# Windowed attention and two expert layers: another order for attention's first steps

## The reference

```
attention (2 batches, 8 heads, 768 positions, 64 wide):
  scores = q k^T / 8;  kept where key < n_sink or 0 <= query - key < window, else -1e9
  a = exp(scores - rowmax);  a /= sum(a) + 1e-9;  x = a v        -> 1536 x 512
expert layer 1: logits = x w_gate + modality_bias[modality_id]; the best of 8 experts per row,
  out = softmax weight * relu(x w1[e]) w2[e]
expert layer 2: all 8 experts, mixed by a table that is normalised over rows and columns 8 times
```

## Time and profile before

| | us |
|---|---|
| median of 3 runs | 1458.73 (1458.69 to 1463.12) |
| profiled execution, its own time | 1461.2 |
| its span | 1459.4 |
| granted TensorE clock, mean | 0.987 |
| PE busy | 1419.9 (97%) |
| DVE, ACT, POOL busy | 515.5, 355.8, 229.6 |
| attention | from 0 to about 149.8 |
| its part in which PE isn't yet without gaps | from 0 to 51.1 |

### The profile page before, as it was taken

The page is one execution under the profiler, slowest core; times in us unless marked ns, Lnnn a source line. Parts: engine busy times, 40 slices in busy tenths (PEclk is TensorE's granted clock), DMA queues, the critical chain, the costliest instruction groups (busy, mean ns, idle before and its releaser), DMA issues.

```text
span 1459.4 us, 18534 instructions
## 1 busy us (share of the span) xinstructions
PE 1419.9 (97%) x7023; PEld 1183.5 (81%) x7024; DVE 515.5 (35%) x935; ACT 355.8 (24%) x627; POOL 229.6 (16%) x252
## 2 busy tenths in 40 slices
PE   8999989999589999999999999999999999999999
PEld 7999678888458888888888888888888888888887
DVE  7887662232453222222222222222222222222222
ACT  4887432322221111121111111121111112121100
POOL 2111022222221111120211111120211111120200
PEclk9999999999799999999999999999999999999999
DMA  5442371121400000000101000000101000010001
GB/s 105 101 96 59 124 260 57 43 101 43 151 29 30 29 29 30 29 29 29 57 0 57 29 29 29 29 29 29 57 0 57 29 29 29 29 34 25 0 20 67
DMA packets 70461, 74.40 MB, mean 51 GB/s; under 512 B 42640, under 2 KB 42640, under 8 KB 70416
## 3 DMA queue, kind: packets, MB, share of 16 engines
q1 hardware_dynamic: 64800, 65.35, 14.2%
q0 software_dynamic: 2576, 8.39, 1.7%
q10 hardware_dynamic: 3040, 0.06, 0.1%
HBM read 63.30 MB, written 10.49 MB: 51 GB/s over the span
## 4 chain that ended last, share of the span: by engine, by line
PE 92%; DVE 4%; issue 2%; DMA 1%; POOL 1%; ACT 0%; SPq 0%; POOLq 0%; DVEq 0%
PE ps L1761 36%; PE ps L1731 35%; PE ps L1629 6%; PE ps L1651 5%; PE ps L1446 2%; PE ps L1375 1%; PE ps L1405 1%; PE ps L1638 1%; PE ps L1563 1%; PE ps L1388 1%; PE ps L1440 1%; PE ps L1360 1%; POOL wsplit L670 1%; DMA v_all<-in_v_dram 1%; PE ps L1609 0%
## 5 line engine op out<-in xcount | busy, mean ns | idle before, releaser
L1731 PE MATMUL ps<-x_hi,wsplit 128*128 128x512 f32 x1536 | 484.1, 390 | 1.4 <-DVE x_lo L1266 1.4
L1761 PE MATMUL ps<-wsplit,h_hi 128*128 128x512 f32 x1536 | 474.6, 390 | 0.0
L1731 PEld LDWEIGHTS ps<-x_hi,wsplit 128*128 128x128 f32 x1536 | 289.1, 188 | 61.6 <-DVE x_lo L1266 1.8
L1761 PEld LDWEIGHTS ps<-wsplit,h_hi 128*128 128x128 f32 x1536 | 289.1, 188 | 59.8
L847 ACT ACTIVATE h_hi<-ps 128x512 fp32r<-128x512 f32 x192 | 114.8, 598 | 866.8 <-PE ps L1731 866.8
L1761 PE MATMUL ps<-wsplit,h_lo 128*128 128x512 f32 x768 | 299.5, 390 | 0.0
L1731 PE MATMUL ps<-x_lo,wsplit 128*128 128x512 f32 x768 | 299.3, 390 | 0.0
L670 POOL TENSOR_TENSOR wsplit<-stage,wsplit 128x2048 fp32r<-128x2048 f32 x32 | 147.1, 4598 | 820.6 <-ACT wsplit L843 820.6
L1289 DVE SCALAR_TENSOR_TENSOR h_lo<-ps,h_hi 128x512 fp32r<-128x512 f32 x192 | 132.7, 691 | 404.9 <-ACT h_hi L847 404.7
L1331 DVE SCALAR_TENSOR_TENSOR acc<-ps,mix,acc 128x512 f32<-128x512 f32 x192 | 143.9, 750 | 347.9 <-PE ps L1761 347.9
L1761 PEld LDWEIGHTS ps<-wsplit,h_lo 128*128 128x128 f32 x768 | 144.6, 188 | 30.1
(11 more groups left out here) (239 smaller groups left out, 979.6 us busy)
## 6 DMA issues: line engine op xcount, KB each, us to landing
stage<-in_moe_w_dram SPq DMA_DIRECT2D x40, 1024.0 KB, 5.2
first_raw<-in_moe_w_dram SPq DMA_DIRECT2D x4, 1024.0 KB, 7.9
q_raw<-in_q_dram SPq DMA_DIRECT2D x12, 256.0 KB, 3.3
k_raw<-in_k_dram SPq DMA_DIRECT2D x12, 256.0 KB, 4.2
v_all<-in_v_dram SPq DMA_DIRECT2D x12, 256.0 KB, 4.6
x_rows_dram<-x_rows SPq DMA_DIRECT2D x12, 256.0 KB, 3.6
y_rows<-y_rows_dram SPq DMA_DIRECT2D x12, 256.0 KB, 4.8
out_dram<-acc SPq DMA_DIRECT2D x12, 256.0 KB, 2.0
```

Source lines behind the costliest of these rows:

```text
L1731: last = pe.matmul(ps[:, f, :], w_part[:, ws], x_part[:, kc, toks], start=(kc == 0 and n == 0), stop=(kc == KD - 1 and n == 2))
L1761: last = pe.matmul(ps[:, 4 + t, :], h_part[:, s % 2, kc, ts], w_part[:, ks], start=(kc == 0 and n == 0), stop=(kc == 3 and n == 2))
```

## The change

It does six things.

1. The six small loads get two semaphores: scalars_loaded for n_sink and window, small_loaded for the other four. DVE waits for the scalars only; the others are waited for where they are used.
2. v gets a semaphore for each tile; a tile's q and k no longer share theirs with v. SP issues q, k of tile 0, the sink keys, q, k of tile 1, then v of both tiles. DVE zeroes v_sink first.
3. DVE makes the masks (with the caps of tiles 0 and 1) before it splits half 0.
4. The sinks' keys are copied once from PSUM into an SBUF table sink_keys, from there in two copies to k_cur (zeroed by a memset), and in four copies to k_sink after masking step 1. POOL waits for these on a semaphore of their own, and copies v of tile 0 first.
5. q and k are transposed, evacuated and split four steps ahead instead of three: a fourth `transpose_qk` and `qk_evacuate` stand in the start, and the loop does step c + 4.
6. In the first iteration, PE transposes step 0's probabilities and runs 8 keep_busy transposes before the scores of step 2; the string before the flag grows from 14 to 20.

```diff
@@ SP
             load_tile(1)
+            load_values(0)
+            load_values(1)
             sp.wait_ge(sinks_zeroed, 1)
...
                 load_tile(m)
+                load_values(m)
@@ POOL, attention_copies
+                def copy_values(t):
+                    pool.wait_ge(v_loaded[2 * i + t], 16)
+                    if not (first_pair and t == 0):
+                        pool.wait_ge(pv_done, lin(i, 4, 2 * t))
+                    hold(2 + t)
+                    pool.tensor_tensor(v_use[:, t, :], v_all_flat[:, bass.ds(lin(i, 2 * DM, t * DM), DM)], ones_row,
+                                       ALU.mult).then_inc(v_ready, 1)
+                if first_pair:
+                    copy_values(0)
...
+                        if first_pair and t == 0:
+                            pool.wait_ge(sinks_copied, 1)
                         pool.wait_ge(scores_done, lin(i, 4, 2 * t + 2))
...
-            pool.wait_ge(sinks_ready, 3)
@@ ACT
-            for c in range(3):
+            for c in range(4):
                 qk_evacuate(0, c)
...
+                    if begin and c == 0:
+                        p_evacuate(i, c)
                     if not (final and c + 1 >= 4):
                         exps(i, c + 1)
-                    if not (final and c + 3 >= 4):
-                        qk_evacuate(i, c + 3)
-                    p_evacuate(i, c)
+                    if not final:
+                        qk_evacuate(i, c + 4)
+                    if not (begin and c == 0):
+                        p_evacuate(i, c)
@@ DVE
+            dve.memset(v_sink[:, :, :, :], 0.0).then_inc(sinks_zeroed, 1)
+            dve.memset(k_cur[:, :, :, :], 0.0).then_inc(k_cur_begun, 1)
...
-            dve.wait_ge(small_loaded, 16 * 6)
+            dve.wait_ge(scalars_loaded, 16 * 2)
             dve.wait_ge(consts_ready, 3)
...
             link(dve.tensor_scalar(sinkcap[:, :, :], sinkcap[:, :, :], KEEP - MASKED, MASKED, ALU.mult, ALU.add))
+            caps(0)
+            caps(1)
+
+            qk_lo(0, 0)
+
+            dve.wait_ge(sinks_ready, 1)
+            dve.tensor_copy(sink_keys[:, :], ps[:, 5, 0:2 * 4 * SINKS]).then_inc(sinks_ready, 1)
+            dve.wait_ge(sinks_ready, 2)
+            dve.wait_ge(k_cur_begun, 1)
+            for h in range(2):
+                rows = slice(h * D, (h + 1) * D)
+                last = dve.tensor_copy(k_cur[rows, :, :, h * SINKS:(h + 1) * SINKS],
+                                       sink_keys[rows, 0:4 * SINKS].rearrange("p (a s) -> p a s", a=HH).unsqueeze(1)
+                                       .to_broadcast([D, 2, HH, SINKS]))
+            last.then_inc(sinks_ready, 1)
+            qk_lo(0, 1)
...
             mask_max(0, 0)
+            qk_lo(0, 2)
+            mask_max(0, 1)
+            sink_evacuate(0, 0)
+            qk_lo(0, 3)
             for b in range(B):
                 for h in range(2):
                     rows = slice(h * D, (h + 1) * D)
+                    last = dve.tensor_copy(k_sink[rows, b * JT // 2:(b + 1) * JT // 2, :, h * SINKS:(h + 1) * SINKS],
...
+            last.then_inc(sinks_copied, 1)
@@ DVE, dve_steps
-                    if not (final and c + 3 >= 4):
-                        qk_lo(i, c + 3)
-                    sink_evacuate(i, c)
+                    if not final:
+                        qk_lo(i, c + 4)
                     if not (begin and c == 0):
+                        sink_evacuate(i, c)
                         x_evacuate(i, c - 1)
@@ PE, scores
+                if i == 0 and c == 0:
+                    pe.wait_ge(sinks_ready, 3)
+                if i == 0 and c == 2:
+                    pe.wait_ge(sinkT_ready, 1)
@@ PE, the start
-            pe.wait_ge(sinks_ready, 2)
             scores(0, 0)
             transpose_qk(0, 2)
             scores(0, 1)
-            keep_busy(14, 4)
+            transpose_qk(0, 3)
+            pe.wait_ge(sinks_ready, 2)
+            keep_busy(20, 4)
@@ PE, pe_steps
+                    if begin and c == 0:
+                        transpose_p(i, c)
+                        pe.wait_ge(masked, 1)
+                        keep_busy(8, 0)
                     if not (final and c + 2 >= 4):
                         scores(i, c + 2)
-                    if not (final and c + 3 >= 4):
-                        transpose_qk(i, c + 3)
-                    transpose_p(i, c, last_masked=(final and c + 2 >= 4))
+                    if not final:
+                        transpose_qk(i, c + 4)
                     if begin and c == 0:
-
                         pe.wait_ge(masked, 2)
                         keep_busy(12, 2)
-                    if not (begin and c == 0):
-                        values(i, c - 1, last_qk=(final and c + 3 >= 4))
+                    else:
+                        transpose_p(i, c, last_masked=(final and c + 2 >= 4))
+                        values(i, c - 1, last_qk=final)
```

More of the change, by code:

```diff
@@ L246, in attention_moe_moe @@
         small_loaded = sem("small_loaded")
-        tile_loaded = [sem("tile_loaded_even"), sem("tile_loaded_odd")]
+        scalars_loaded = sem("scalars_loaded")
+        tile_loaded = [sem("qk_loaded_even"), sem("qk_loaded_odd")]
+        v_loaded = [sem(f"v_loaded{m}") for m in range(TILES)]
+        sinks_copied = sem("sinks_copied")
+        k_cur_begun = sem("k_cur_begun")
         sinks_loaded = sem("sinks_loaded")
@@ L407, in load_tile, with load_values @@
                 b, rows = m // JT, slice((m % JT) * PART, (m % JT + 1) * PART)
-                for src, dst in ((q, q_raw[:, m % 2, :]), (k, k_raw[:, m % 2, :]), (v, v_all[:, m, :])):
+                for src, dst in ((q, q_raw[:, m % 2, :]), (k, k_raw[:, m % 2, :])):
                     sp.dma_start(dst.rearrange("p (h d) -> p h d", h=H),
                                  src[b, :, rows, :].rearrange("h s d -> s h d")).then_inc(tile_loaded[m % 2], 16)
+            def load_values(m):
+                b, rows = m // JT, slice((m % JT) * PART, (m % JT + 1) * PART)
+                sp.dma_start(v_all[:, m, :].rearrange("p (h d) -> p h d", h=H),
+                             v[b, :, rows, :].rearrange("h s d -> s h d")).then_inc(v_loaded[m], 16)
             load_tile(0)
@@ L929, in qk_lo @@
                                   ks_hi[:, 2 * half:2 * half + 2, par, :], ALU.subtract).then_inc(qk_split, 1)
-            qk_lo(0, 0)
-            dve.wait_ge(sinks_ready, 1)
-            for par in range(2):
-                for h in range(2):
-                    rows = slice(h * D, (h + 1) * D)
-                    dve.tensor_copy(k_cur[rows, par, :, (1 - h) * SINKS:(2 - h) * SINKS],
-                                    k_sink[rows, 0, :, (1 - h) * SINKS:(2 - h) * SINKS])
-                    last = dve.tensor_copy(k_cur[rows, par, :, h * SINKS:(h + 1) * SINKS],
-                                           ps[rows, 5, 0:4 * SINKS].rearrange("p (a s) -> p a s", a=HH))
-            last.then_inc(sinks_ready, 1)
-            qk_lo(0, 1)
             link(dve.tensor_scalar(okj[:, :, :], rel[:, :, :], scal[:, 1:2], None, ALU.is_lt))
@@ L1001, in _ @@
                     rows = slice(h * D, (h + 1) * D)
-                    src = ps[rows, 5, b * 4 * SINKS:(b + 1) * 4 * SINKS].rearrange("p (a s) -> p a s", a=HH)
-                    for i in range(JT // 2):
-                        last = dve.tensor_copy(k_sink[rows, b * JT // 2 + i, :, h * SINKS:(h + 1) * SINKS], src)
-            last.then_inc(sinks_ready, 1)
-            qk_lo(0, 2)
-            mask_max(0, 1)
-            caps(1)
+                    last = dve.tensor_copy(k_sink[rows, b * JT // 2:(b + 1) * JT // 2, :, h * SINKS:(h + 1) * SINKS],
+                                           sink_keys[rows, b * 4 * SINKS:(b + 1) * 4 * SINKS]
+                                           .rearrange("p (a s) -> p a s", a=HH).unsqueeze(1)
+                                           .to_broadcast([D, JT // 2, HH, SINKS]))
+            last.then_inc(sinks_copied, 1)
             def dve_steps(i, begin=False, final=False):
@@ L1408, in transpose_p @@
                 pe.wait_ge(sinks_packed, lin(i, 4, c + 1))
-                if not last_masked:
+                if i == 0 and c == 0:
+                    pe.wait_ge(sinks_masked, 2)
+                elif not last_masked:
                     pe.wait_ge(sinks_masked, lin(i, 4, c + 3))
```

34 lines of the change are left out of this document (14 added, 20 removed).

## The result

| | before | after |
|---|---|---|
| median (lowest to highest), 20 runs each | 1460.85 (1458.69 to 1463.34) | 1458.56 (1456.28 to 1460.06) |
| profiled execution: time, span, clock | 1461.2, 1459.4, 0.987 | 1458.2, 1456.4, 0.990 |
| step 3's masking, scores of step 7, of step 8 | 31.35, 51.08, 56.21 | 27.98, 47.09, 53.21 |
| last x_rows | 149.38 | 145.91 |

The ratio is 0.9981, 95% interval [0.9974, 0.9987]: 2.8 us less (1.9 to 3.8), or 2.3 by the medians. The forecast was 4.8 us less. The sign held, but the time came out above the range of 1451.7 to 1457.8. Part of that is the base: the forecast subtracted from 1458.73, the median of three runs, and 20 runs have theirs at 1460.85. Moved up by these 2.12 us, the range would have held the result; the forecast itself, 1460.85 - 4.8, would still be 2.5 too low.

What follows compares the result with a forecast made beforehand. DVE was taken to bound the first 51 us, PE the rest. Terms of -3.6 to step 3's masking, -0.7 in steps 3 to 7 and -0.5 at attention's end gave -4.8: 1458.73 to 1453.9, range 1451.7 to 1457.8.

Steps and rivals of the forecast that it cites:

- Steps 3 to 7: After step 3's masking: PE's remaining waits hide in DVE's length, DVE's 0.68 idle goes; -0.7, -4.3 in all.
- Own semaphore for the scalars: In the start, DVE begins the scalars at 5.85 instead of 9.47: -3.6 us.
- Masks ahead of q and k: In the start, masks and caps fill DVE's wait for q and k; the 0.34 idle goes, range 0 to -0.3.
- v's own semaphores: In the start, PE could begin 0.87 earlier but DVE comes last; no gain alone, about 0.3 lost without them.
- The walk itself: Step-by-step timing of the start: DVE idle 0.4 before step 0's masking, step 3's masking at 27.7 against 31.35.
- PE order in step 0: Step 0's probabilities' transposes and 8 fillers stand before step 2's scores, so DVE waits: +0.6.
- The end of attention: One set of four transposes moves from the stretch that PE bounds into the start: -0.5.
- The clock: PE's longest gap, 18.4 to 19.75, was expected to leave the granted clock at 1.00 from 9 to 100 us.
- rival A: Clock falls once near 19 to 22 us for about 7 us; gain 2.1 to 2.8, about 1456.2; chance 0.12.
- the rule on transposes: Trainium skill: transposes don't count as busy for the clock; by it the clock falls between 16 and 21.6 us.
- rival C: The clock keeps falling in attention's steps; 15 to 20 us of low clock give +2 to +3, 1461.3; chance 0.06.
- Rival D: Low-clock stretches behind 186 us and in 438 to 474 shift; 1 to 1.5 us either way, counted as width, no chance given.

Runs made afterwards that it cites:

- e2: Changed kernel with GpSimd's copy of v's tile 2 waiting for DVE's fourth x_rows; last x_rows 145.27, ratio to the kernel before 0.9986.
- g1: Changed kernel whose DVE again waits for all six small loads before making the scalars; last x_rows 153.07, ratio to the kernel before 1.003.
- r1: The changed kernel run and profiled again, unchanged; last x_rows 146.24, median 1457.96, ratio to the kernel before 0.9984.
- e1: Changed kernel with GpSimd's copy of v's tile 0 waiting for DVE's first masking; last x_rows 145.67, ratio to the kernel before 0.9983.
- d3: Changed kernel with step 0's probabilities transposed behind step 2's scores again, without the 8 fillers; last x_rows 145.13, ratio to the kernel before 0.9977.
- d2: Kernel before with only the q/k transposes, evacuations and splits a step further ahead; last x_rows 149.40, ratio to the kernel before 1.0009.
- e4: Changed kernel without the 8 filling transposes ahead of step 2's scores; last x_rows 145.49, ratio to the kernel before 0.9981.
- d1: Kernel before with only the separate semaphores (scalars, v) and the masks first; last x_rows 146.55, median 1459.47, ratio to the kernel before 0.9998.
- f1: Changed kernel with GpSimd's copy of each tile of v in four instructions instead of one; last x_rows 147.93, ratio to the kernel before 0.9986.
- h2: d4 with 36 instead of 48 warm-up transposes on PE; last x_rows 145.04, median 1454.08, ratio to the kernel before 0.9951.
- h3: Changed kernel with 60 instead of 48 warm-up transposes on PE; last x_rows 149.77, ratio to the kernel before 0.9998.
- d4: d3 with GpSimd's copies of v's tiles 0 and 2 held back as in e3; last x_rows 144.09, median 1455.1, ratio to the kernel before 0.9969.
- r2: d4 run and profiled again, unchanged; last x_rows 144.53, median 1455.88, ratio to the kernel before 0.9967.
- h1: Changed kernel with 36 instead of 48 warm-up transposes on PE; last x_rows 145.89, median 1456.83, ratio to the kernel before 0.9973.
- j1: d5 with 36 instead of 48 warm-up transposes on PE; last x_rows 143.93, median 1455.53, ratio to the kernel before 0.9964.
- e3: Changed kernel with both of GpSimd's copies (v's tiles 0 and 2) held back, as in e1 and e2; last x_rows 145.05, ratio to the kernel before 0.9978.
- d5: d4 with GpSimd's copy of v's tile 1 also waiting for x_rows; last x_rows 145.05, median 1455.47, ratio to the kernel before 0.9968.

## Why the prediction was wrong

Attention gained 3.47 us where 4.8 were forecast. Of the 1.33 that are missing, 0.23 were lost up to step 3's masking (3.37 for 3.6), 0.08 from there to the scores of step 7 (0.62 for 0.7), 0.99 from the scores of step 7 to those of step 8, and 0.03 at the end (0.47 for 0.5). By the forecast's own steps:

*Steps 3 to 7* is the step that failed. It ended with what PE waits for being "the attention output of two steps back, some 0.3 a step, hidden in DVE's own length". Up to the scores of step 7 this is nearly so: 3.99 gained (51.08 to 47.09) where 4.3 were forecast. But from step 7 to 8 PE took 6.12 us instead of 5.13. e2 shows that GpSimd's second copy makes 0.56 of it there (0.64 by the last x_rows). Without that copy the sinks' scores of step 8 still stand 5.57 behind those of step 7 (48.00 and 53.57), where the kernel before has 5.13. In these 0.44, PE's transposes of q follow the sinks' scores by 0.69 instead of 0.47, and the three pieces behind its transposes of the probabilities each start 0.05 to 0.1 late. They lie where the bound passes from DVE to PE, right behind DVE's x_rows and masking. That DVE is what PE waits for there is read from this order and was not tested.

The forecast had no term for GpSimd's copies of v. They cost because they moved against DVE's work: in the kernel before rden started at 51.15, just ahead of the copy at 51.23. The Trainium skill ("GPSIMD Engine Reference", 1. Specifications) says that GpSimd shares its SBUF interfaces with VectorE and contends with DVE instructions in a 2-port mode or with two SBUF inputs. The runs agree for the split, which has two SBUF inputs (1.30 for 0.42). rden and the mask table have one, and no run shows in which mode they run; they were held too (0.94 for 0.17, 1.39 for 0.50). By that sentence the copies would have been a term of the sum, and it was not used.

*Own semaphore for the scalars*: right. The scalars come 3.80 earlier for the 3.6 forecast, and g1 shows that without it nothing is left. The terms up to step 3 add to 3.44, the text took 3.6, and 3.37 were measured.

*Masks ahead of q and k*, with *v's own semaphores* called cover: "DVE is what comes last", with PE's warm-up ending at 8.8. That is right for the first split, but step 0's masking follows the first q by 5.20 from 8.5 or so on. The walk itself had this in its 0.4 of idle (8.8 + 5.2 is its 14.0), and the sentence didn't say it. r1, with the first q at 9.06, had gained only 3.04 at step 3. So 8.8 was one execution's value of something that varies by over a microsecond. The agreement at step 0 in the first profile, 14.20 for 14.0, is part luck: the warm-up ended 0.4 earlier than assumed, and the copy of v gave that back. e1's 0.24 for this copy holds for an early warm-up; in r1 the copy came at 13.08, held nothing, and step 0 was masked at 14.26 all the same.

*PE order in step 0*: the idles were sized rightly (0.94 and 0.63 for 0.9 and 0.6), and the sum contained them. That they could be avoided was not asked: d3 masks step 2 two microseconds sooner at equal warm-up, and ends attention 1.1 sooner.

*The end of attention*: right, 0.47 for 0.5 (the scores of step 8 came 3.00 earlier, the last x_rows 3.47).

*The clock*: it stayed at 1.00 up to 146 us in both profiles of the changed kernel; rival A did not occur in them. Whether the new order keeps it there is less sure, for d2 kept it too with PE's long waits still in its start. Against the rule on transposes stand now the rows of the changed kernel from 18.5 to 21.6, e4, and g1, where PE ran only transposes from 22.49 to 29.26 and the granted clock rose from 0.50 to 1.00 meanwhile. Something like rival C exists in small: in the profiles of d1, g1, f1, h2 and h3 the clock fell once within attention, at 1.1 us of cost in h2 and 1.6 in h3. Behind attention h3 has another 2.7 us, a gap of 1.34 and transposes at half pace (2.81 for 1.48 us at 150.66).

*Rival D, the stretches behind attention*, was counted as width, and rightly. The granted clock there in some profiles, with the time from the last x_rows to the end of the span:

| | 180:196 | 360:400 | 400:450 | rest |
|---|---|---|---|---|
| before | 0.79 | 0.79 | 0.93 | 1310.0 |
| after | 0.89 | 0.74 | 0.97 | 1310.5 |
| after again (r1) | 0.79 | 0.79 | 0.93 | 1310.7 |
| d4 again (r2) | 0.89 | 0.79 | 0.93 | 1309.2 |
| d4, h1, h2, j1 | 0.89 | 0.83 | 0.93 | 1308.3, 1307.8, 1307.8, 1307.6 |

Two executions of the changed kernel differ in all three, so they belong to the execution and not to the program, as r1's expectation had it in its second half; the 0.5 us that it wanted for the rest did not follow (0.2). In this table the rest is shorter, by up to 3 us, where the clock in 360 to 400 is higher, but these clocks don't settle it: e4 has 0.89, 0.74 and 0.93 with a rest of 1310.8, f1 the clocks of h1 with 1308.0, and h3, with its gap, the same clocks and 1311.3. Of the 3.47 that attention gained, 0.5 went there in the first profile. Some 0.4 of that has its own row: the transposes of x_rows at 145.29 took 1.84 instead of 1.48 (in r1 and e3 a gap of 0.41 with "issue" among them); before, h1, r2 and d4 don't have it. What causes it stays open.

One sum of the range was off as well: the low end's 2.2 us are, by the bounds that the text gives, 0.3 for the copies, 0.17 for DVE's start and 1.5 for D, so 2.0. It changes nothing, for the result lies beyond the other end.

## What to carry to other kernels

When work is moved in time, list which DVE instructions each GpSimd copy will now meet. A GpSimd instruction of a microsecond can hold a tiny DVE instruction until it ends. A wait on the right event avoids that at no cost that was seen (e2, e3), and a wait on the wrong event only moves the hold to the next DVE instruction of that kind (d5, j1): check it in the trace. When the wait that came last goes, look at how much the next one varies between executions, not at its value in one profile, and compare two profiles at equal starts. And take a forecast's base from many runs: here 3 runs were 2.1 us off, nearly as much as the change brought.

## What the runs showed of the hardware

- Some DVE instructions are held while a 1.04 us GpSimd copy runs: a subtraction of two SBUF inputs of 128x256 (1.30 instead of 0.42), an fp32 addition of a constant on 128x4 elements (0.94 to 1.04 instead of 0.15), and two fp32 instructions of 128x256 with constants (1.39 instead of 0.50). With copies a quarter as long the first two took 0.68 and 0.37. Others beside a copy kept their length: a reciprocal of 128x4 (0.18 at 51.33 in the kernel before) and the masking with a PSUM input (1.22 at 48.74 in e2).
- The change from the slow to the fast pace of PE after its first matmul comes at different times: 48 transposes took 6.85 to 8.29 us over the profiles, at a granted clock of 1.00 throughout.
- With nothing but transposes on PE the granted clock stayed at 1.00 after 1.5 us of idling (changed kernel, 20.02 to 21.60), and rose from 0.50 in 22 to 26 us to 0.82 in 26 to 28 and 1.00 in 28 to 30 (g1).
- Equal waits were followed by a fall in one execution and not in another: with PE busy 1.13 of 2 us the clock fell to 0.50 in h3 (50 to 52) and stayed at 1.00 in r1 (48 to 50). It fell to 0.57 in 15 to 18 us behind a wait of only 1.04 us in d1, and not behind one of 2.09 us in d2.
